# Pooled attention and two feed-forward layers on one core: weight sums moved from GpSimd to VectorE, splits in pairs, attention steps spaced out

## The reference

```python
k_p = k.reshape(B, H, Sp, pool, D).mean(axis=3)      # pool 8, Sp 72
v_p = v.reshape(B, H, Sp, pool, D).mean(axis=3)
scores = scale * np.matmul(q, k_p.transpose(0, 1, 3, 2))
attn = softmax(scores)                               # over the 72 pooled keys
x = np.matmul(attn, v_p)                             # to [4608, 512]
h = x @ w_in; r = np.maximum(h, 0.0); g = s * (r * r) + b
x = g @ w_out                                        # 512 -> 2048 -> 512
h = x @ w_in2; g = h / (1.0 + np.exp(-h))
out = g @ w_out2
```

## Time and profile before

| | us |
|---|---|
| median of 3 runs | 1815.12 |
| lowest, highest | 1812.32, 1815.92 |
| the profiled execution: time | 1824.48 |
| its span | 1822.7 |
| TensorE, VectorE, ScalarE, GpSimd busy | 90%, 68%, 47%, 22% of the span |

### The profile page before, as it was taken

The page is one execution under the profiler, slowest core; times in us unless marked ns, Lnnn a source line. Parts: engine busy times, 40 slices in busy tenths (PEclk is TensorE's granted clock), DMA queues, the critical chain, the costliest instruction groups (busy, mean ns, idle before and its releaser), DMA issues.

```text
span 1822.7 us, 30205 instructions
## 1 busy us (share of the span) xinstructions
PE 1648.2 (90%) x11926; PEld 1621.4 (89%) x11926; DVE 1244.0 (68%) x1494; ACT 859.4 (47%) x1232; POOL 405.6 (22%) x422
## 2 busy tenths in 40 slices
PE   7887679669989999999989999899989999899999
PEld 6877579569989999899989999898989999899999
DVE  7476646737768676777768586776767687675765
ACT  4343444335554445545455445545455455544443
POOL 5576766532011110202012110201111020100000
PEclk8888889889999999999999999999999999999999
DMA  5666677489979998899979998798988999799997
GB/s 168 211 228 237 250 256 283 178 316 315 324 260 349 328 326 294 280 379 314 329 252 352 341 318 298 257 395 286 334 285 283 359 318 320 259 361 344 332 330 263
DMA packets 155740, 542.80 MB, mean 298 GB/s; under 512 B 17104, under 2 KB 17104, under 8 KB 153552
## 3 DMA queue, kind: packets, MB, share of 16 engines
q1 hardware_dynamic: 151248, 531.43, 82.1%
q10 hardware_dynamic: 4352, 9.44, 1.3%
HBM read 464.39 MB, written 76.41 MB: 297 GB/s over the span
## 4 chain that ended last, share of the span: by engine, by line
PE 66%; DVE 13%; DMA 9%; POOL 6%; ACT 3%; issue 3%; SPq 0%; ACTq 0%; DVEq 0%; POOLq 0%
PE a_ps L770 19%; PE b_ps L770 14%; PE a_ps L748 14%; PE b_ps L748 10%; DMA xa_dram<-probs 3%; DMA w_dram<-w_stage 3%; PE t_ps L624 2%; POOL w_stage L561 2%; DVE gq L1164 2%; PE t_ps L637 2%; DVE ring L1115 2%; DVE probs L1091 1%; DVE rowsum L1083 1%; DVE gq L1171 1%; DMA ring<-w_dram 1%
## 5 line engine op out<-in xcount | busy, mean ns | idle before, releaser
L748 PE MATMUL a_ps<-xc_hi,ring 128*128 128x288 f32 x1792 | 409.6, 305 | 19.0 <-DMA ring<-w_dram 15.4
L770 PE MATMUL a_ps<-sp_hi,ring 128*128 128x288 f32 x1792 | 369.1, 295 | 0.7 <-DMA ring<-w_dram 0.7
L748 PEld LDWEIGHTS a_ps<-xc_hi,ring 128*128 128x128 f32 x1792 | 308.4, 194 | 22.2 <-issue 15.6
L748 PE MATMUL b_ps<-xc_hi,ring 128*128 128x288 f32 x1344 | 301.5, 299 | 5.3 <-DVE gq L1164 5.3
L770 PEld LDWEIGHTS a_ps<-sp_hi,ring 128*128 128x128 f32 x1792 | 291.3, 188 | 1.3 <-DMA ring<-w_dram 1.3
L1213 DVE TENSOR_TENSOR sp_lo<-gq,sp_hi 128x1152 fp32r<-128x1152 f32 (+1 forms) x182 | 199.4, 1108 | 136.1 <-ACT sp_hi L927 135.5
L770 PE MATMUL b_ps<-sp_hi,ring 128*128 128x288 f32 x1344 | 276.8, 295 | 0.0
L748 PE MATMUL a_ps<-xc_lo,ring 128*128 128x288 f32 x896 | 269.6, 301 | 0.0
L770 PE MATMUL a_ps<-sp_lo,ring 128*128 128x288 f32 x896 | 264.5, 295 | 0.0
L748 PEld LDWEIGHTS b_ps<-xc_hi,ring 128*128 128x128 f32 x1344 | 229.1, 191 | 6.7 <-DVE gq L1164 6.7
L927 ACT ACTIVATE sp_hi<-gq 128x1152 fp32r<-128x1152 f32 (+1 forms) x182 | 169.0, 940 | 131.8 <-PE b_ps L770 62.7
(11 more groups left out here) (156 smaller groups left out, 2856.8 us busy)
## 6 DMA issues: line engine op xcount, KB each, us to landing
ring<-w_dram SPq DMA_DIRECT2D x784, 512.0 KB, 5.2
w_dram<-w_stage SPq DMA_DIRECT2D x64, 512.0 KB, 5.8
w_dram<-ring SPq DMA_DIRECT2D x48, 512.0 KB, 2.9
w_raw<-weights SPq DMA_DIRECT2D x16, 1024.0 KB, 6.8
out<-yb ACTq DMA_DIRECT2D x16, 576.0 KB, 6.5
k_stage<-kT SPq DMA_DIRECT2D x30, 288.0 KB, 4.0
q_sb<-qT SPq DMA_DIRECT2D x30, 288.0 KB, 4.7
v_stage<-vP SPq DMA_DIRECT2D x30, 288.0 KB
```

The costliest lines, as they stand in the source:

```text
L748: last = nc.tensor.matmul(bank[:, half, 0:th], w, xc_of(x, th)[:, j, k, :], start=(first and k == 0 and i == 0), stop=(k == 1 and i == 2), ...
L770: last = nc.tensor.matmul(bank[:, m, 0:th], w, split_of(g, th, turn, 2 * c + half), start=(first and half == 0 and i == 0), stop=(end and ...
```

## The change

- VectorE takes over the four sums of a set (one in each of slots 0 to 3) and their low parts (slots 5 and 7). GpSimd keeps only attention's pooling.
- Roundings and low parts, of quadrants and of sums, are made two granules at a time: slots 0 and 2 of a set for the quadrants, 4 and 6 for the sums' roundings. w_stage has two places of two granules, and a store of sums moves two granules. Semaphore values follow.
- `down_banks` is in another order, t_ps last; the waits on its eviction follow, as do those of the first Strassen products and of the attention jobs on these banks.
- Attention's steps lie at offsets 0, 1, 2, 3, 4, 6, 7, 9, 10, 12, 13, 15, 16 of a job's start (SPACED), and for the job that spans the border of up and down at OVER_EDGE. Jobs start at 0, 17, 64 and 81 in the plain stage, and at 0, 19, 40 and 58 of a unit.

```diff
-STAGE = 3
+STAGE = 2
...
-FIRST_TURNS = (0, 15, 64, 80)
-TURN_SLOTS = (0, 14, 58, 72)
+SPACED = (0, 1, 2, 3, 4, 6, 7, 9, 10, 12, 13, 15, 16)
+OVER_EDGE = (0, 1, 2, 3, 4, 6, 7, 9, 12, 15, 16, 18, 19)
+FIRST_TURNS = ((0, SPACED), (17, SPACED), (64, SPACED), (81, SPACED))
+TURN_SLOTS = ((0, SPACED), (19, OVER_EDGE), (40, SPACED), (58, SPACED))
...
-    ("prep", 1), ("lo0", 2), ("lo1", 2), ("lo0", 3), ("lo1", 3), ("prep", 2), ("prep", 3), ("values", 2), ("values", 3),
+    ("prep", 1), ("lo0", 2), ("lo1", 2), ("lo0", 3), ("lo1", 3), ("values", 2), ("values", 3),
 ]
-FIRST_GPSIMD = [("values", 0), ("values", 1), ("keys", 2), ("keys", 3), ("values", 2), ("values", 3), ("set", 0)]
+FIRST_GPSIMD = [("values", 0), ("values", 1), ("keys", 2), ("keys", 3), ("values", 2), ("values", 3)]
...
-        w_stage = sb("w_stage", [P, STAGE, GRAN], F32R)
+        w_stage = sb("w_stage", [P, STAGE, 2, GRAN], F32R)
...
-        down_banks = ((t_ps, a_ps[1], b_ps, a_ps[0]), (t_ps, b_ps, a_ps[0], a_ps[1]))
+        down_banks = ((a_ps[1], b_ps, a_ps[0], t_ps), (b_ps, a_ps[0], a_ps[1], t_ps))
...
             def load_set(q):
                 if q >= 2:
-                    sp.wait_ge(f_wlo, 4 * (q - 2) + 4)
+                    sp.wait_ge(f_wlo, 2 * (q - 2) + 2)
                     sp.wait_ge(f_sum, 4 * (q - 2) + 4)
...
-                if i >= 4:
-                    store_sum(q, i - 4)
+                if i in (5, 7):
+                    store_sum(q, i // 2 - 2)
...
-                if i == 0 and q:
-                    sum_set(q)
-                if i >= 4:
-                    low_sum(q, i - 4)
...
                     elif t == PAIRS + 2:
-                        pe.wait_ge(f_xlo, PAIRS + 1)
+                        pe.wait_ge(f_xlo, 2 * PAIRS)
...
+            def sum_set(q, n):
+
+                a11, a12, a21, a22 = [w_raw[:, q % 2, i, :] for i in range(4)]
+                s1, s2 = w_sum[:, 0, :], w_sum[:, 1, :]
+                if n == 0:
+                    dve.wait_ge(raw_landed[q % 2], (q // 2 + 1) * DMA)
+                    left, right = a21, a22
+                    if q:
+                        dve.wait_ge(f_slo, 2 * q)
+                else:
+                    dve.wait_ge(f_sum, 4 * q + n)
+                    left, right = ((s1, a11), (a12, s2), (a11, a21))[n - 1]
+                nc.vector.tensor_tensor(w_sum[:, n, :], left, right, ALU.subtract if n else ALU.add).then_inc(f_sum, 1)
+
+            def low_sum(q, n):
+                done = by_pair(w_stage[:, (2 * q + n) % STAGE, :, :])
+                dve.wait_ge(f_whi, sum_split(q, n))
+                nc.vector.tensor_tensor(done[:, :, 1, :], sum_pair(n), done[:, :, 0, :].bitcast(F32),
+                                        ALU.subtract).then_inc(f_slo, 1)
...
-                if i < 4 and q + 1 < SETS:
-                    prep_plain(q + 1, i)
+                if i in (0, 2) and q + 1 < SETS:
+                    prep_plain(q + 1, i // 2)
+                if i < 4:
+                    sum_set(q, i)
+                elif i in (5, 7):
+                    low_sum(q, i // 2 - 2)
```

More of the change, by code:

```diff
@@ L117, in schedule @@
         assert upto - t <= len(slots)
-        for base, job in zip(slots, range(t, upto)):
-            for i, name in enumerate(TURN_NAMES):
+        for (base, offsets), job in zip(slots, range(t, upto)):
+            for i, name in zip(offsets, TURN_NAMES):
                 table[s, base + i] = (name, job)
@@ L240, in flat, with by_pair @@
             return bank[:, :, :].rearrange("p b n -> p (b n)")
+        def by_pair(granules):
+            return granules.rearrange("p g (h l n) -> p (g h) l n", h=2, l=2)
         def halves(row):
             return row.rearrange("p (b n) -> p b n", b=2)
-        def by_chunk(granule):
-            return granule.rearrange("p (h l n) -> p h l n", h=2, l=2)
         hi_flat = sp_hi[:, :, :].rearrange("p s n -> p (s n)")
@@ L349, in values_done, with plain_split, plain_pair, raw_pair @@
             return t + 1 if t < PAIRS else PAIRS + 2 * (t - PAIRS) + e + 1
-        def plain_split(q, m):
-            return m + 1 if q == 0 else 8 * q - 4 + m + 1
+        def plain_split(q, n):
+            return n + 1 if q == 0 else 4 * q - 2 + n + 1
         def sum_split(q, n):
-            return 8 * q + (8 if q < SETS - 1 else 4) + n + 1
+            return 4 * q + (4 if q < SETS - 1 else 2) + n + 1
         def set_stored(q, j):
             if 1 <= j <= 4:
-                n = 4 * q + j - 1
+                n = 2 * q + (j - 1) // 2
                 return s_stored[n % STAGE], (n // STAGE + 1) * DMA
             return r_stored[(4 * q + {0: 0, 5: 1, 6: 3}[j]) % RING], (q // 2 + 1) * DMA
+        def plain_pair(q, n):
+            first = (4 * q + 2 * n) % RING
+            return by_pair(ring[:, first:first + 2, :])
+        def raw_pair(q, n):
+            return w_raw[:, q % 2, 2 * n:2 * n + 2, :].rearrange("p a (h n) -> p (a h) n", h=2)
+        def sum_pair(n):
+            return w_sum[:, 2 * n:2 * n + 2, :].rearrange("p a (h n) -> p (a h) n", h=2)
         def piece_used(n):
@@ L416, in store_sum @@
             def store_sum(q, n):
[L417 to L420, removed]
+                (done, _), row, step = set_stored(q, 1 + 2 * n), row_of_set(q, 1 + 2 * n), 1 if q % 8 < 4 else 4
+                sp.wait_ge(f_slo, 2 * q + n + 1)
+                sp.dma_start(w_dram[row:row + step + 1:step].rearrange("j p n -> p j n"),
+                             w_stage[:, (2 * q + n) % STAGE, :, :].bitcast(F32)).then_inc(done, DMA)
             def sets_of(ph, slot):
@@ L541, in pool_values @@
                 pool.wait_ge(v_used, t + 1)
[L543 to L560, removed]
-                nc.gpsimd.tensor_tensor(done[:, :, 1, :], halves(w_sum[:, n, :]), done[:, :, 0, :].bitcast(F32),
-                                        ALU.subtract).then_inc(f_slo, 1)
             def attention(turn, t):
@@ L572, in _ @@
                     pool_keys(n)
-                elif turn == "values":
+                else:
                     pool_values(n)
-                else:
-                    sum_set(n)
             pool_keys(PAIRS)
             for slot in range(FSLOTS):
-                q, i = divmod(slot, PLAIN)
-                if i == 0 and q:
-                    sum_set(q)
-                if i >= 4:
-                    low_sum(q, i - 4)
                 attention(*turn_at(-1, slot))
```

59 lines of the change are left out of this document (28 added, 31 removed).

## The result

| | before | changed |
|---|---|---|
| median | 1815.5 us | 1714.2 us (1710.9 to 1719.1, 4 runs) |
| ratio | | 0.9446, 95% interval 0.9418 to 0.9474 |
| span of the profiled execution | 1822.7 | 1713.9 |
| first plain product starts (us from the span's start, here and below) | 50.7 | 42.1 |
| first Strassen product starts | 385.9 | 297.8 |

The change made the kernel 101 us faster; 140 us were forecast. The spans of the two profiled executions differ by more, 108.8 us, since the profiled execution of before was 9 us above its median and that of the changed kernel 1.4. By stage, the span's gain is 8.6 us in the preamble, 79.5 in the plain stage (335.2 to 255.7) and 20.7 in the six units with attention.

The account below looks back on a forecast made before the run. Staging slots, GpSimd's operations and stores were taken to bound the plain stage, mostly products with attention stalls the phases; 1824.5 - 3 - 79 - 60 = 1682.5, less 9.4 to the median, gave 1675 us, range 1640 to 1745.

Parts of the forecast that it names:

- rival 2: Plain stage: the raw load loop sets the set's period at 18 us; 1712 us in all, chance 0.16.
- Start: Preamble: set 0's sums leave GpSimd and paired preps let the next key load issue sooner; -3 us, bounds 0 and -5.7.
- VectorE's load in the plain stage: VectorE takes GpSimd's sums and low parts, and its other operations stretch less: 219 us busy, from 199.8.
- Rival 4: Plain stage: VectorE becomes the bound because its operations keep their price; 1857 us, decides from 1.12 us per 512 columns, chance 0.05.
- Staging at no cost: w_stage: a rounding waits for a store about 11 us before, against 7.7 us a store, so hidden; cost zero.
- Plain stage: Before the Strassen phases: transfers at 92% of their best, 249 us, plus 7 at the end; 256 against 335, -79.
- raw load's loop: Plain stage: raw weights load in 6.6 us, used 6.4 us later; ScalarE and VectorE sit 1 or 2 us, TensorE unaffected.
- end wait: End of the plain stage: TensorE waits for its first granules 7 us in place of 15.4.
- Bank order: Plain down stages, t_ps last: third job's scores wait once for the first layer's last low part, about 2 us, bounds 0 and 4.
- Spacing: Six attention units: more lead per waiting step and a job moved to the even down stage; -60 us, bounds 0 and -85.
- Rival 1: Even down stage is full: the moved job pushes VectorE's low parts past TensorE's need; 1733 us, chance 0.19.
- Sum: Whole kernel: 1824.5 - 3 - 79 - 60 = 1682.5 us, less 9.4 is 1673; stated as 1675 us.

Follow-up runs that it names:

- start experiment: Kernel before, with only the four sums of set 0 moved from GpSimd's preamble to slot 0 of the plain stage: 1814.9 us, ratio 0.9984.
- jobs apart: Changed kernel with the third and fourth attention jobs of a unit started at slots 43 and 63 in place of 40 and 58: 1693.3 us, ratio 0.9319.

## Why the prediction was right, and where its size was off

The time, 1714, lies in the range of 1640 to 1745, the sign is right, and so is the cause of the larger part, w_stage's loop and GpSimd's sums in the plain stage; the gain is 72% of the forecast. It is outside the forecast's own range of 1645 to 1705. It lies next to rival 2's 1712, but not by rival 2's sum: that has 40 us from the plain stage and 60 from the units, and measured are 79.5 and 20.7. Of the signs named, the first Strassen product (297.8 for 305), pairs (1.22 us) and w_stage's stores came as said; sums took 0.69 for 0.6, transfers ran at 309 GB/s for above 310, and a unit with attention took 205.5 us for 198.

- *Start*, -3 (bounds 0 and -5.7): measured -8.6, outside its bounds. The bound was wrong in kind: TensorE's 5.69 us of idle time before scores are what a faster load can save only if TensorE's preamble ahead of it stays as it was; VectorE's steps ahead of it came earlier too. The start experiment puts 2.5 to 6 us on GpSimd's sums.
- *VectorE's load in the plain stage*, 219 us: measured 205.9. Pairs at 1.16 us took 1.22 in the median, and the new work took 125 us in place of 115 (38.6, 38.9 and 47.8 us for pairs, low pairs and sums); but its other operations fell from 120.6 to 80.6 us, where 103.6 were left in the forecast. Rival 4 falls: a sum's 0.69 us is far below 1.12.
- *Staging at no cost*: right, 7.3 us of waits are left of 112. As the old kernel with four places shows, the store's loop alone was worth 40 of 79.5 us, and ScalarE's waits for raw loads stand right behind it.
- *Plain stage*, 256 us with the end: measured 255.7, but that is luck, since it was not for the reason given. The forecast's 249 us came from bytes at 92% of the best rate, and with half the granules' bytes the stage still takes 241.5. What TensorE lost is idle time of 30.5 us (all idle times over 0.3 us of its weight loads; 95.4 before) and the lower clock around it, on work of 216 us. In this trace all of it stands before attention's steps and before the first Strassen product: 9.3 us before turn0, 12.9 before scores, 4.5 before value steps, 3.9 at the end. (In two of the four other traces of the same code one product of the second down stage waited 2.7 and 2.9 us for weights too.) Spacing is worth 15 us there. The raw load's loop was named, and held to be hidden from TensorE. For the products it was: they ran at 12.7 us a set while the loop took 14.0 and 14.4. It reached TensorE by another way, which the prediction did not have: it made VectorE late with the last low part of the layer, for which scores wait. With loads shorter or earlier, in three kernels, that wait is 1.8 us in place of 4.4. The end wait was 3.6 us, and 7 were forecast.
- *Bank order*: TensorE waited 4.2 us once for the last low part of the first layer before scores, just above the bound of 4, and 2 were forecast; the 1.8 us of the kernels with earlier loads are near that. The prediction counts it as a new cost, but the scores waited at this place before as well, 5.5 us for the first of these low parts (L1149, above). A second wait that was not forecast, of 6.2 us, is scores of the first job of the units for VectorE's copy out of t_ps, which is last now. The order was not tried by itself.
- *Spacing*, -60 (bounds 0 and -85): measured -20.7 in the traces. This is the term that was mis-sized, by 39 us; the start gave 6 of them back. The stalls in the up stages went as worked out: 5 us in an even one and 12 in an odd one. The step that failed is the moved job's: "I leave 2 us of stall for it" looked at the store of its result and at VectorE's sum of work, 45 of 49 us, and not at what t_ps waits for. VectorE had 43.5 us of work in a stage that became 57 long; each of four steps came late by its place in the queue, and one wait cost the clock as well. The same slots in the kernel before give the same loss, 57 to 61 us. Rival 1 had the place right and its mechanism wrong: TensorE never waited there for a low part of the products, and with the third job's steps moved on (39.4 us of VectorE's work left) the stage takes 48.0 us.
- *Sum*: -8.6 - 79.5 - 20.7 = -108.8 against -3 - 79 - 60 = -142 for the profiled executions.

## What to carry over

When a step moves in a hand-written order, list for it what the step waits for on every engine, the PSUM bank's last reader included, and what stands ahead of that reader in its own queue; an engine that is 80% busy on the average can be 2 us late at the one place that counts. Before an engine is made faster, look at the reuse distance of the buffer it fills: one more place was worth 40 us of the plain stage by itself here. Then look at the next loop behind the one that is opened, and at TensorE's own waits: a loop longer than TensorE's work (14.0 us a set against 12.7) can stay hidden from its products and still reach it through one step at the end of a layer. And of steps that several engines hand around, leave the lead where the slowest queue has its burst.

## What the runs showed of the hardware

TensorE's granted clock fell to half for some 14 matmuls, 3 us, behind an idle time of 2.0 us before scores (changed kernel's row at 578.18) and one of 2.7 us before turn0 (second of the earlier trace rows). In the kernel with jobs apart it did not behind 2.7 us before the first value step in the second unit, and did behind 2.8 us before the same step in the third. So the length of the idle time alone does not tell it. VectorE's operation on 10 columns (L1085) took 1.07 us while GpSimd summed, and 0.45 without. 1 MB loads of raw weights landed in 4.7 to 10.0 us in the changed kernel's plain stage; with granules of half the bytes the median went from 5.6 to 5.1 us only, but in the first down stage from about 7 to 5.0.
